# Linear attention in halves of 64 tokens, every attention matmul on a 64x64 part of the array

## The reference

```python
for t in range(S):
    kt, vt, rt = (k[:, :, t], v[:, :, t], r[:, :, t])
    cur = np.einsum('bhd,bhe->bhde', u[None] * kt, vt)
    y[:, :, t] = np.einsum('bhd,bhde->bhe', rt, state + cur)
    state = w[None, :, :, None] * state + np.einsum('bhd,bhe->bhde', kt, vt)
...
g = x @ w_gate
silu = g * (1.0 / (1.0 + np.exp(-g)))
val = x @ w_val
return (silu * val @ w_out).astype(np.float32)
```

## Time and profile before

| | us |
|---|---|
| median of 3 runs | 1065.5 (1064.79 to 1066.11) |
| the profiled execution | 1063.25 |
| its span on the core | 1061.5 |
| TensorE busy | 1029.3 |
| VectorE busy | 565.0 |
| GpSimd busy | 480.7 |
| ScalarE busy | 342.1 |

### The profile page before, as it was taken

How to read it: one execution, slowest core, us unless ns; L and a number is a source line. 1 busy time by engine, 2 the same in 40 slices (tenths; PEclk the granted TensorE clock), 3 DMA queues, 4 the chain that set the end, 5 groups by cost and what they waited for, 6 DMA issues and landing times.

```text
span 1061.5 us, 21081 instructions
## 1 busy us (share of the span) xinstructions
PE 1029.3 (97%) x8732; PEld 865.2 (82%) x8732; DVE 565.0 (53%) x712; ACT 342.1 (32%) x689; POOL 480.7 (45%) x385
## 2 busy tenths in 40 slices
PE   3799999999999999999999999999999999999997
PEld 3689998888888888888888888888888888888886
DVE  8999996675666667666235624315225234234110
ACT  2354343333333333433243431222321312312211
POOL 7789886664555566565133322122222222222121
PEclk9899999999999999999999999999999999999999
DMA  5553432222322132232042210000100100100000
GB/s 216 189 197 103 150 124 93 68 68 68 103 99 97 43 122 68 68 97 69 4 149 89 90 60 1 30 31 1 60 1 1 60 1 1 60 1 1 31 0 30
DMA packets 23982, 72.75 MB, mean 69 GB/s; under 512 B 4624, under 2 KB 7760, under 8 KB 23888
## 3 DMA queue, kind: packets, MB, share of 16 engines
q1 hardware_dynamic: 23888, 71.41, 20.1%
HBM read 60.87 MB, written 9.44 MB: 66 GB/s over the span
## 4 chain that ended last, share of the span: by engine, by line
PE 93%; DVE 3%; POOL 2%; issue 1%; ACT 0%; ACTq 0%; DVEq 0%; POOLq 0%
PE ps_val L420 10%; PE ps_down L420 9%; PE ps_gate L420 9%; PE ps_down L422 9%; PE ps_down L421 9%; PE ps_val L422 9%; PE ps_val L421 9%; PE ps_gate L421 9%; PE ps_gate L422 9%; PE ps_level L484 5%; PE ps_y L515 2%; PE ps_y L537 2%; DVE r_level L789 1%; PE ps_level L496 1%; POOL pair_prod L1010 1%
## 5 line engine op out<-in xcount | busy, mean ns | idle before, releaser
L980 POOL TENSOR_TENSOR h_lo<-h_raw,h_hi 128x512 fp32r<-128x512 f32 (+1 forms) x156 | 211.4, 1355 | 465.2 <-ACT h_hi L609 465.1
L761 DVE TENSOR_TENSOR h_raw<-h_raw,ps_val 128x512 f32<-128x512 f32 (+1 forms) x156 | 100.8, 646 | 423.7 <-PE ps_val L422 423.3
L609 ACT ACTIVATE h_hi<-h_raw 128x512 fp32r<-128x512 f32 (+1 forms) x156 | 93.5, 599 | 296.6 <-DVE h_raw L761 296.4
L420 PE MATMUL ps_val<-x_hi,val_hi 128*128 128x512 f32 (+1 forms) x468 | 177.9, 380 | 3.6 <-DVE h_raw L761 3.5
L420 PE MATMUL ps_gate<-x_hi,gate_hi 128*128 128x512 f32 (+1 forms) x468 | 178.7, 382 | 1.3 <-ACT down_hi L620 1.3
L420 PE MATMUL ps_down<-h_hi,down_hi 128*128 128x512 f32 (+1 forms) x468 | 175.9, 376 | 1.0 <-issue 1.0
L603 ACT ACTIVATE h_raw<-ps_gate 128x512 f32<-128x512 f32 (+1 forms) x156 | 88.0, 564 | 270.1 <-PE ps_gate L422 268.7
L422 PE MATMUL ps_val<-x_lo,val_hi 128*128 128x512 f32 (+1 forms) x468 | 174.9, 374 | 0.0
L421 PE MATMUL ps_val<-x_hi,val_lo 128*128 128x512 f32 (+1 forms) x468 | 174.9, 374 | 0.0
L421 PE MATMUL ps_gate<-x_hi,gate_lo 128*128 128x512 f32 (+1 forms) x468 | 174.8, 374 | 0.0
L422 PE MATMUL ps_gate<-x_lo,gate_hi 128*128 128x512 f32 (+1 forms) x468 | 174.8, 374 | 0.0
(11 more groups left out here) (87 smaller groups left out, 1162.5 us busy)
## 6 DMA issues: line engine op xcount, KB each, us to landing
r_block<-in_r_blk_dram SPq DMA_DIRECT2D x24, 768.0 KB, 4.6
staging<-in_weights_dram SPq DMA_DIRECT2D x36, 384.0 KB, 3.7
chunk_in<-in_a_t_dram SPq DMA_DIRECT2D x24, 512.0 KB, 3.6
chunk_in<-in_a_n_dram SPq DMA_DIRECT2D x24, 384.0 KB, 4.8
chunk_in<-x_dram SPq DMA_DIRECT2D x6, 768.0 KB, 5.6
out_dram<-x_out SPq DMA_DIRECT2D x6, 768.0 KB, 4.0
x_dram<-x_out SPq DMA_DIRECT2D x5, 768.0 KB, 7.0
x_raw<-y_last SPq DMA_DIRECT2D x132, 8.0 KB, 2.8
```

What stands on the lines that cost most here:

```text
L420: nc.tensor.matmul(dst, w_hi, x_h, start=first, stop=False)
L609: nc.scalar.activation(h_hi[:, f % 3, 0:WIDTH[t]], h_raw[:, f % 2, 0:WIDTH[t]], ACT.Copy).then_inc(h_hi_done, 1)
L761: nc.vector.tensor_tensor(h_raw[:, f % 2, 0:WIDTH[t]], h_raw[:, f % 2, 0:WIDTH[t]], ps_val[:, 0:WIDTH[t]], ALU.mult)\
L980: nc.gpsimd.tensor_tensor(h_lo[:, f % 3, 0:WIDTH[t]], h_raw[:, f % 2, 0:WIDTH[t]], h_hi[:, f % 3, 0:WIDTH[t]].bitcast(F32), ALU.subtract). ...
```

## The change

A chunk is still loaded and scaled as 128 tokens, but its scores are computed within halves of 64 only. Level 4, which joined the halves, is gone; what the second half needs of the first comes through the state, which is now passed from half to half.

- Levels: `LEVELS` is 4; all have 16 matmuls of 64x64 weights on 32 columns. `a_mat` holds for each head a 128x64 matrix (two halves one above the other), so `take_low` is one instruction per level instead of two, and `take_block` covers 512 elements instead of 1024.
- State: `state_in` (before the chunk, double buffered) and `state_mid` (before its second half). `sums` makes two contributions, one per half. On VectorE `decay_mid`, `sum_mid` and `sum_end` do decay, add, decay, add. `spread_state` and its copies on ScalarE are gone.
- `carried`, `own`, `sums`: 16 matmuls each where there were 8, each with a weight tile of at most 64x64 and 64 (or 48) columns. Consecutive ones go to the four quarters of the array. `carried` is in two parts (turn 0 and 1) with levels 0 to 2 of the next chunk between.
- Banks: the result of a chunk lies in `ps_val`, bank 0 of which is the value product's. So TensorE waits for `h_done` before turn 0, and the next val slot waits for `y_copied`.
- Chunks 0 and 1, ahead of the MLP: `sums(1)` and `for_sums(1)` come ahead of their results, chunk 0 has its own `for_carried`, and `copy_last`, `fill` and `copy_first` take the place of the tail tricks (`fill_v_tail`, `fill_state_tail`). Memsets and the last step of the power table go. One table of 256 KB (`turns`) is loaded.
- Slots: `LOW_AT` is now 1, 15, 27 in tile 0 and 35 (the last slot), then 9, 18 and 27 after the start of the next tiles; before it was 1, 12, 27 and then 4, 12, 20, 28 of each tile. `HIGH_AT` is 0.6 of the way to the next. Level 3 and `sums` stand there.

```diff
-LEVELS = 5
+LEVELS = 4
...
+EARLIEST = (1, 15, 27)
+EVERY = (-1, 9, 18, 27)
+LOW_AT = {2 + _j: _s for _j, _s in enumerate(EARLIEST)}
+for _t in range(1, TILES1 - 1):
+    for _j, _s in enumerate(EVERY):
+        LOW_AT[FIRST[_t + 1] + 1 + _j] = _t * SLOTS + _s
+UPPER = 0.6
+HIGH_AT = {_g: LOW_AT[_g] + int((LOW_AT[_g + 1] - LOW_AT[_g]) * UPPER) for _g in range(2, NCH)}
...
+MULTIPLY, DECAY, TAKE_LOW, SUM_STATE = (0.2, 0.2), 0.1, (0, 0.4), 0.2
+SUM_PAIRS, TAKE_BLOCK, SCALE_R = (0.45, 0.45), 0.4, (0.4, 0.97, 0.97, 0.97)
+TAKE_THIRD = 0.4
+FOR_CARRIED, FOR_SUMS, WEIGH, SCALE_K = 0.6, 0.1, (0.55, 0.95), (0, 0.7, 0.7, 0.77)
...
+        ps_val = ctx.enter_context(nc.psum_tensor("ps_val", [P, 2, BANK], F32))
...
+        def result_out(g, half):
+            if g == 1:
+                return ps_down[:, 2, 0:HP * HALF] if half else ps_gate[:, 0:HP * HALF]
+            return ps_val[:, half, 0:HP * HALF]
...
+                        for half in range(1 if g % CPB == CPB - 1 else 2):
+                            rows = slice(half * HALF, (half + 1) * HALF)
+                            place = slot * HP + hp
+                            last = nc.tensor.matmul(sums_out(g, half)[slot * SLOT:slot * SLOT + D, hp, :], k_state[rows, place, :],
+                                                    v_n(g)[rows, place, :], start=True, stop=True)
...
-            def carried(g):
...
+            def carried(g, turn):
...
+                if turn == 0:
                     pe.wait_ge(block_in, g + 1)
...
+                    pe.wait_ge(r_state_done, g + 1)
+                    sums_taken(pe, g)
+                    if g >= SIZES[0]:
+                        reach(pe, y_copied, g)
...
+                    pe.wait_ge(y_begun, g + 1)
...
+                            if half == 0 and g and g % CPB == 0:
+                                continue
+                            hp = 2 * side + n
+                            rows = slice(slot * SLOT, slot * SLOT + D)
+                            before = state_mid[rows, hp, 0:width] if half else state_in[rows, g % 2, hp, 0:width]
+                            at = (slot * 2 + n) * HALF
+                            last = nc.tensor.matmul(result_out(g, half)[side * SLOT:side * SLOT + width, at:at + HALF], before,
+                                                    r_state[rows, hp, half * HALF:(half + 1) * HALF],
+                                                    start=(g, side, half) not in begun, stop=False, skip_group_check=True)
+                            begun.add((g, side, half))
+                if turn == 0:
+                    last.then_inc(y_begun, 1)
...
             def own(g):
...
+                for slot in range(2):
+                    for n in range(2):
+                        for side in range(2):
+                            for half in range(2):
+                                rows = slice(half * HALF, (half + 1) * HALF)
+                                place = slot * HP + 2 * side + n
+                                at = (slot * 2 + n) * HALF
+                                last = nc.tensor.matmul(result_out(g, half)[side * SLOT:side * SLOT + D, at:at + HALF],
+                                                        v_n(g)[rows, place, :], a_of(g)[rows, place, :],
+                                                        start=(g, side, half) not in begun, stop=True, skip_group_check=True)
+                                begun.add((g, side, half))
...
-            for l in range(LOW, LEVELS):
-                level(0, l)
-            sums(0)
+            level(0, LOW)
             for l in range(LOW):
                 level(1, l)
-            own(0)
-            for l in range(LOW, LEVELS):
-                level(1, l)
-            carried(1)
-            own(1)
+            sums(0)
+            level(1, LOW)
+            sums(1)
+            for g in range(SIZES[0]):
+                carried(g, 0)
+                carried(g, 1)
+                own(g)
+                fill(g)
...
-                                result(g - 1)
-                            else:
-                                sums(1)
+                                pe.wait_ge(h_done, h_before(t, s))
+                                carried(g - 1, 0)
                             for l in range(LOW if g < NCH else 0):
                                 level(g, l)
+                            if g > 2:
+                                carried(g - 1, 1)
+                                own(g - 1)
                         if g < NCH and HIGH_AT[g] == t * SLOTS + s:
-                            for l in range(LOW, LEVELS):
-                                level(g, l)
+                            level(g, LOW)
+                            sums(g)
...
+                act.wait_ge(low_in, (LOW - 1) * (g + 1))
...
+            def take_high(g):
+                if g < SIZES[0]:
+                    act.wait_ge(level_done, LEVELS * g + LEVELS)
+                else:
+                    act.wait_ge(sums_done, g + 1)
...
+                nc.vector.copy_predicated(by_slot(a_of(g)).rearrange("p s h (b x l) -> p s h b x l", x=2, l=L)[:, :, :, :, 1, :],
...
+            def decay_mid(g):
+                if g % CPB != 0:
+                    dve.wait_ge(state_done, updates(g - 1))
+                    reach(dve, y_done, g)
+                    decays[0] += 1
+                    nc.vector.tensor_tensor(state_mid[:, :, 0:D], state_in[:, g % 2, :, 0:D], over_half, ALU.mult).then_inc(state_decayed, 1)
+            def sum_mid(g):
+                dve.wait_ge(sums_done, g + 1)
+                dve.wait_ge(high_in, g + 1)
+                if g == 0:
+                    dve.wait_ge(state_zero, 2)
                 if g % CPB == 0:
-                    reach(dve, state_done, updates(g - 1))
-                    nc.vector.tensor_copy(kept, ps_state).then_inc(state_summed, 1)
+                    reach(dve, y_done, g)
+                    nc.vector.tensor_copy(state_mid[:, :, 0:D], sums_out(g, 0)).then_inc(mid_done, 1)
...
+                    dve.wait_ge(state_decayed, decays[0])
+                    nc.vector.tensor_tensor(state_mid[:, :, 0:D], state_mid[:, :, 0:D], sums_out(g, 0), ALU.add).then_inc(mid_done, 1)
+            def sum_end(g):
+                if g % CPB != CPB - 1:
+                    after = state_in[:, (g + 1) % 2, :, 0:D]
+                    dve.wait_ge(mid_done, g + 1)
+                    reach(dve, y_done, g)
+                    decays[0] += 1
+                    nc.vector.tensor_tensor(after, state_mid[:, :, 0:D], over_half, ALU.mult).then_inc(state_decayed, 1)
+                    dve.wait_ge(state_decayed, decays[0])
+                    nc.vector.tensor_tensor(after, after, sums_out(g, 1), ALU.add).then_inc(state_done, 1)
...
+                        if late_spot(g, SUM_STATE) == at:
+                            sum_mid(g)
+                            sum_end(g)
```

In the val slot of `group` stands one more wait:

```diff
+                    reach(pe, y_copied, results(t * SLOTS + ORDER.index(("val", f))))
```

410 lines of the change are left out of this document (173 added, 237 removed).

## The result

The changed kernel takes 1053.9 us (median of 4 runs, 1053.35 to 1057.27) against 1065.2 us before (4 runs on the same chip), a ratio of 0.990 (95% interval 0.988 to 0.992). The forecast was 1038.5 us with a range of 1029 to 1052: the direction was right, less than half of the gain came, and the time lies outside the range. The profiled execution took 1057.27 us, with a span of 1055.2; the other three had spans of 1051.3 to 1052.5, so some 3 us of what follows belong to this one execution.

A forecast was written before the change was run, and what follows sets the result against it. TensorE was taken to bound the wide tiles, VectorE tile 0, both tile 1. Terms of -22 (wide tiles), -1 (tiles 0 and 1) and -3 (start) took 1065.5 to 1039.5, one more microsecond to 1038.5 us; range 1029 to 1052.

The forecast's parts named there:

- TensorE in a wide tile: Tiles 2 to 5: a chunk costs 3.93 us instead of 5.08, at 16 ns per record; 22 us less.
- I put these waits at nothing: Wide tiles: new waits around results, val slots and VectorE's products just fit, so they add nothing.
- Tiles 0 and 1: Narrow tiles before the wide ones: about 62 and 57 us, together -1 us.
- So tile 0 should take about 62 us: Tile 0: VectorE sets the pace and gets more chunk work, so about 62 us instead of 60.4.
- If tile 0 takes over 66 us, my count of VectorE's work was wrong: Sign for tile 0 in the profile after: over 66 us would mean VectorE's work was miscounted.
- Rival C: New waits in most chunks, 0.5 us each, or tile 0 at its upper bound: +8 to +11, 1048 us, chance 0.16.
- ends: Tiles 0 and 1 together: -8 us without any wait, +7 if TensorE waits 1 us in each of seven down slots.
- The start: Before the first MLP matmul, which comes at about 37.5 instead of 40.5 us: -3, between -5 and +1.
- the last microsecond of the forecast: Taken off 1039.5 to give 1038.5 us, since carried, sums, own and levels now share one shape.
- Rivals B and D: Price of a new record: B 25 ns, 1056 us, chance 0.10; D 35.6 ns, 1076 us, chance 0.05.
- C: Theory of the experiments, not the prediction's rival: in tiles 0 and 1 hand-offs between engines, each waiting in turn, cost the time.
- L: Rival theory of the experiments, not in the prediction: the load of VectorE or GpSimd sets tiles 0 and 1.

The follow-up runs named there:

- e10: Changed kernel, with levels 0 to 2 placed one slot later, apart from the preceding carried and own, at chunks 10, 13, 15 and 20 only: 1046.0 us.
- e2: Changed kernel, with levels 0 to 2 of every next chunk moved one slot later, behind the following gate product; take_low and scale_k of level 0 too: 1055.9 us.
- e17: Kernel of e10, with the runs of chunks 3 and 5 (tile 0's two issue stalls) parted too: 1047.5 us.
- e12: Kernel before the change, old form of attention, with one more chunk's worth of attention placed in tile 0: 1068.4 us.

## Why the prediction was wrong

- **TensorE in a wide tile: right, and a little too dear.** A chunk was to cost 3.93 us. Without stops and partings tiles 2 to 5 take 350.9 us (e10) where 353.5 were forecast, 2.6 less or 0.17 a chunk: the records cost 14 to 15 ns where 16 were taken.
- **"I put these waits at nothing", wide tiles: right as far as waits for data go,** and wrong for what was not on the list. Packing 88 records closer made a run of 160 records in 2.5 us out of 144 in 3.9, and the fetch of the program showed: +8.6 us. Before, no wait of TensorE is named in these tiles.
- **Tiles 0 and 1: the step that failed.** "So tile 0 should take about 62 us", and tile 1 57 "with small waits": the length was taken from VectorE's work, because it had been busy for 57.8 of 60.4 us before. The count of that work was right (58.96 us busy), the waits were not. The prediction's own sign ("If tile 0 takes over 66 us, my count of VectorE's work was wrong") reads this falsely. Tile 0 took 69.6, tile 1 62.1: 12.7 us more than forecast. Some 3 to 4 of them may belong to this execution, and in e10, with the same program there, the tiles took 126.2. TensorE was idle for 15.3 of the 131.7 us: 5.1 in stops for the program, which the prediction did not have at all, 8.5 in waits for results, 1.5 unnamed. The stops are not the whole of it: where tile 0 had none of them (e2, e17) both tiles still took 126.1 and 126.5 us, with more a_mat waits, 7 us above the forecast. Rival C named the waits for data, with an upper bound of +7 for both tiles against the kernel before; they grew by 11.5. In the "ends" I had priced waits only for the short down slots.
- **The start:** 39.0 in place of 37.5; no run here asks why.
- The terms together: 1.5 + 12.7 + 6.0 (8.6 - 2.6) = 20.2 us on the span; the profiled execution of after lies 3.35 us above its median and that of before lay 2.25 below its own, which leaves 14.6 of the 15.4 us by which the forecast missed. Most of the rest is the last microsecond of the forecast, taken off for one shape of records, which the cheaper records above already hold.
- **Rivals B and D:** refuted by 14 and 15 ns a record.

Open: what sets tiles 0 and 1 at 126 us and more once the stops are away. That hand-offs do it (C) is argued from the waits that come back and from the failure of L, and not shown; five reorderings and two relieved engines did not free these tiles, and no run took the extra chunk out of them altogether.

## What to carry to other kernels

When work is packed closer, ask what feeds it: for TensorE also the program, 16 KB a piece. Look for "issue" in the waits, count the records between the stops and the packets of the program's queue in the same windows, and see whether each stop ends the same time after a packet. Then part the run that is hit, and only that one, since parting has its own price (here 0.72 us). An engine that is 95% busy does not tell what one more piece of work costs on it: price the hand-offs of that piece as well. Moving it in the old kernel first (e12) is cheap and warned of the longer tile; but look at the busy times beside the length, since there it was VectorE's work that grew.
